# Both magnitude sums of the second expert's w2b ahead of tile 1's Relu, and 26 of 30 early w1a pieces beside the attention chunks

## What is computed

```python
# attention: B=4, H=8, S=768, D=64, gamma per head
state = gamma * state + k_t v_t^T
y_t = scale * q_t @ state
x = y as [3072, 512]
# soft MoE (phi, w1a, w2a): 4 slots per expert
logits = x @ phi
slot_in = softmax(logits, axis=0).T @ x
slot_out[e] = relu(slot_in[e] @ w1a[e]) @ w2a[e]
x = softmax(logits, axis=1) @ slot_out
# top-2 MoE (w_gate, w_noise, noise, w1b, w2b)
noisy = x @ w_gate + log1p(exp(x @ w_noise)) * noise
for each token, its two best experts e with weights p:
    out += p * relu(x @ w1b[e]) @ w2b[e]
```

## Time and profile before

| | us |
|---|---|
| median of 3 runs | 539.45 (538.11 to 540.13) |
| the profiled execution | 539.68 |
| its span | 537.8 |
| PE busy | 492.4 (92%) |
| DVE, ACT, POOL busy | 276.2, 185.8, 254.2 |

### The profile page before, as it was taken

One profiled execution on the slowest core, in us unless ns is written; L12 is line 12 of the kernel. 1 busy time (PEld: TensorE's weight loads), 2 busy tenths in 40 slices (PEclk: granted clock), 3 DMA queues, 4 the chain that ended last, 5 costly groups with the idle time before them and its releaser, 6 DMA issues.

```text
span 537.8 us, 13565 instructions
## 1 busy us (share of the span) xinstructions
PE 492.4 (92%) x4844; PEld 291.5 (54%) x4845; DVE 276.2 (51%) x443; ACT 185.8 (35%) x346; POOL 254.2 (47%) x217
## 2 busy tenths in 40 slices
PE   3999999987978667989999999999999999999995
PEld 3877787863567243444544544545545445445452
DVE  2676766666221897463646455464545332433422
ACT  0222222221003537665455363554442222223210
POOL 2222222202000024525777868786878766666553
PEclk9999999998997889999999999999999999999999
DMA  7999999989999999342466342132232332433410
GB/s 276 400 359 398 401 401 404 380 340 333 403 425 424 390 417 400 112 174 85 161 217 198 102 137 49 27 58 45 44 59 44 53 47 43 57 42 42 60 20 2
DMA packets 35096, 107.93 MB, mean 201 GB/s; under 512 B 11871, under 2 KB 13135, under 8 KB 32624
## 3 DMA queue, kind: packets, MB, share of 16 engines
q1 hardware_dynamic: 20880, 92.90, 44.6%
q0 software_dynamic: 14176, 14.49, 14.8%
HBM read 93.87 MB, written 29.43 MB: 229 GB/s over the span
## 4 chain that ended last, share of the span: by engine, by line
PE 76%; DMA 13%; DVE 3%; issue 3%; POOL 2%; ACT 1%; SPq 1%; DVEq 0%; POOLq 0%
PE ps L1019 47%; DMA w_region<-moe_w 7%; PE ps L1002 4%; PE ps L672 4%; PE ps L736 4%; DMA late_w1a<-chunks 4%; PE ps L856 3%; PE ps L885 3%; DMA out<-s_region,rec_region 2%; PE ps L712 2%; PE ps L726 2%; PE ps L747 2%; PE ps L686 1%; POOL out L625 1%; SPq L524 1%
## 5 line engine op out<-in xcount | busy, mean ns | idle before, releaser
L1019 PE MATMUL ps<-w_region,s_region 128*128 (+1 forms) x1304 | 290.4, 379 | 2.0 <-DVE s_region L1704 1.0
L1019 PEld LDWEIGHTS ps<-w_region,s_region 128*128 128x128 f16 x1304 | 125.4, 98 | 143.4 <-issue 2.8
L1674 DVE SCALAR_TENSOR_TENSOR s_region<-ps,s_region 128x1024 f16<-128x1024 f32 x55 | 67.3, 1224 | 144.2 <-ACT s_region L1232 144.1
L1232 ACT ACTIVATE s_region<-ps 128x1024 f16<-128x1024 f32 x55 | 56.3, 1024 | 176.5 <-PE ps L1002 176.5
L619 POOL DMA_INDIRECT out<-s_region,rec_region x41 | 53.9, 1315 | 49.4 <-DVE s_region L1704 46.1
L625 POOL DMA_INDIRECT out<-s_region,rec_region x42 | 66.9, 1593 | 19.2 <-issue 11.9
L613 POOL DMA_INDIRECT rec_region<-records,idx x55 | 60.1, 1092 | 24.4 <-issue 16.3
L559 POOL TENSOR_TENSOR s_region<-w_region,s_region 128x512 f32<-128x512 f32 x14 | 14.6, 1043 | 50.0 <-PE ps L747 31.9
L1002 PEld LDWEIGHTS ps<-s_region,sw_region 128*128 (+1 forms) x440 | 29.6, 98 | 14.0 <-issue 0.8
L1704 DVE TENSOR_SCALAR s_region<-ps,rec_region,y_scale 128x512 f32<-128x512 f32 x42 | 33.8, 805 | 5.9 <-PE ps L1019 4.1
L1002 PE MATMUL ps<-s_region,sw_region 128*128 128x128 f16 x440 | 34.5, 219 | 0.5 <-ACT s_region L1227 0.4
(11 more groups left out here) (249 smaller groups left out, 571.1 us busy)
## 6 DMA issues: line engine op xcount, KB each, us to landing
w_region<-moe_w SPq DMA_DIRECT2D x49, 512.0 KB, 11.2
w_region<-moe_w SPq DMA_DIRECT2D x10, 2048.0 KB, 8.7
w_region<-chunks SPq DMA_DIRECT2D x26, 512.0 KB, 7.2
s_region<-moe_w SPq DMA_DIRECT2D x4, 2048.0 KB, 12.9
sw_region<-chunks SPq DMA_DIRECT2D x12, 512.0 KB, 7.2
late_w1a<-chunks SPq DMA_DIRECT2D x8, 512.0 KB, 8.2
w_region<-moe_w SPq DMA_DIRECT2D x3, 1024.0 KB, 8.0
s_region<-moe_w SPq DMA_DIRECT2D x5, 512.0 KB, 8.4
```

What stands on the lines that cost most here:

```text
L1019: last = nc.tensor.matmul(bank[6 + r], h[:, r, f, :], w2b_parts[:, bass.ds(o, 1), part, f, :].rearrange("p e m -> p (e m)"), start=(first ...
L1232: nc.scalar.activation(h_hi[:, r, :, :].rearrange("p c t -> p (c t)").rearrange("p (a n) -> p a n", a=2), ps[:, 2 + 2 * r:4 + 2 * r, :], A ...
L1674: nc.vector.scalar_tensor_tensor(out=h_lo[:, r, :, :].rearrange("p c t -> p (c t)").rearrange("p (a n) -> p a n", a=2), in0=ps[:, 2 + 2 * ...
```

## The change

Two things are changed. First, only 26 pieces of w1a are issued beside the chunks. After chunk g there are g - 2 of them up to chunk 10, and from chunk 11 on one more for every third chunk. The other four (quarters 2 and 3 of expert 6, quarters 0 and 1 of expert 7) follow behind the noise, ahead of the wait for x_t, with a semaphore of their own, for which L856 waits at expert 6.

Second, both sums of the second expert's w2b follow each other on ACT, ahead of ct of tile 2 and the Relu of tile 1. The reduction stands on POOL after the sixth fetch, and the scale on DVE ahead of the low part and y of tile 1 and 0.

```diff
+        CHUNK_QUARTERS = EARLY_QUARTERS - 4
...
-                more = (g - 2) * EARLY_QUARTERS // (NT - 3)
+                more = g - 2 + max(0, g - 8) // 3
                 for q in range(ahead, more):
-                    w1a_quarter(q // 4, q % 4)
+                    w1a_quarter(q // 4, q % 4, w1a_early)
...
             sp.dma_start(noise_t, noise[:, :, :]).then_inc(noise_full, 16)
+            for q in range(CHUNK_QUARTERS, EARLY_QUARTERS):
+                w1a_quarter(q // 4, q % 4, w1a_late)
             sp.wait_ge(x_t_ready, NT)
...
-            for i in range(4, 2 * DEPTH + 3):
+            for i in range(4, DEPTH + 2):
+                fetch_records(i)
+            w2b_all_sum(EARLY)
+            for i in range(DEPTH + 2, 2 * DEPTH + 3):
                 fetch_records(i)
...
-                if i == 0:
-                    w2b_all_sum(EARLY)
...
-            pe.wait_ge(w1a_early, 16 * EARLY_QUARTERS)
+            pe.wait_ge(w1a_early, 16 * CHUNK_QUARTERS)
             for e in range(E):
+                if e == CHUNK_QUARTERS // 4:
+                    pe.wait_ge(w1a_late, 16 * (EARLY_QUARTERS - CHUNK_QUARTERS))
...
-            w2b_sum_part(EARLY, 0, junk)
             stage_c(2, 0, rec_arrival(2))
+            w2b_sums(EARLY, junk)
+            keep_ct(2, 0)
             h_high(1, 1)
-            keep_ct(2, 0)
             stage_c(3, 1, rec_arrival(3))
+            keep_ct(3, 1)
             h_high(2, 0)
-            keep_ct(3, 1)
-            w2b_sum_part(EARLY, 1, junk)
             w2b_high(EARLY)
...
-            low_keep(0, 0, None)
-            h_low(2, 0)
             w2b_scale_by_sum(EARLY)
             dve.wait_ge(order_ready, 1)
             scale_y(EARLY)
+            low_keep(0, 0, None)
+            h_low(2, 0)
             w2b_low(EARLY)
```

7 lines of the change are left out of this document (4 added, 3 removed).

## The result

| | us |
|---|---|
| before, median of 20 runs | 539.7 (536.6 to 541.59) |
| after, median of 20 runs | 542.55 (538.26 to 545.69) |
| ratio | 1.0051, 95% interval 1.0035 to 1.0067 |
| the profiled execution of after | 541.53, span 539.6 |

The change costs 2.8 us where 4.1 us of gain were forecast. The kernel after was timed twice more, each time against before on the same chip: 1.0021 (0.9989 to 1.005) and 1.005 (1.0013 to 1.0086). The profiled executions differ by 1.85 us (541.53 - 539.68). In the kernel after, lines ahead of the second MoE's tile loop are 5 to 7 higher (L1019 is L1026, L1476 is L1482, L1485 is L1491, L928 is L935, L856 is L863, L672 is L677), and on POOL 4 higher (L619 is L623, L625 is L629, L589 is L593).

A forecast was written before the change was run, and what follows sets the result against it. The prediction saw full DMA bounding the kernel until the last w1b piece, then PE in the tile loop. From the profiled 539.68 us, -3.0 (A) and -1.1 (B) gave 535.6, as a median 535.4; range 533.8 to 538.8.

The forecast's parts named there:

- Part A: Moving four w1a pieces behind the noise: fewer chunk waits and a filled DMA hole, -3.0 us, bounds -3.5 and -1.0.
- (a): Attention: with fewer w1a pieces ahead of the chunks, all 3.0 us of PE's avoidable chunk waits go, lower end 2.0.
- (c): Early attention, one piece per chunk: landings of 5.8 us stay above 3.2, so no new DMA idle time.
- (b): DMA at 119 to 128 us: four moved pieces (2.1 MB, 5.4 us) fill a hole of 3.2 us; L856 starts at 126.0.
- Rival (1): Front: the queue drains before chunk 10, up to 3.9 us idle replaces the hole's 3.2; 538.3 us, chance 0.14.
- Part B: Reordered start of the tiles: -0.55 at tile 3 and -0.55 at the second PE wait, -1.1 us, bounds -2.0 and +2.4.
- the first wait: PE's 0.99 us wait for y of tile 1 before tile 3, forecast to go: start at 234.5 instead of 235.01.
- The hold of POOL: POOL's DMAs slowed beside DVE's low halves of expert 1: at worst tile 1's rows go out 0.75 us later.
- rival (3): Tiles: POOL holds DVE, two waits of at most 1.6 us, y of tile 1 at 235.1; 536.0 us, chance 0.06.
- So ACT starts at 248.1 to 248.5: ACT on expert 2's high half starts 0.8 to 1.2 us earlier; PE waits about 0.5 us instead of 1.00.
- rival (2): Tile 0's rows land behind the w2b[3] load, expert 2's scale is late, PE loses 2.4 us; 538.8 us, chance 0.16.
- (5): Fuller DMA queues cause more untraced waits, read as code fetches, on DVE or PE; 541.0 us, slower, chance 0.07.

The follow-up runs named there:

- front_only: Only the w1a part of the change (26 pieces beside the chunks, four behind), tiles in the old order, against before: 546.33 us, ratio 1.002.
- tiles_sum2_w2b3_late: Before plus the new tile order, the third expert's w2b reduction ahead of tile 2's add, and w2b[3] loaded after tile 5's Relu: 536.89 us, 0.9933.
- tiles_sum2_early: Before plus the new tile order and the third expert's w2b reduction ahead of tile 2's add: 537.11 us, 0.9944; run again 537.64 us, 0.987.

## Why the prediction was wrong

**Part A, -3.0 forecast, -0.24 in the profile.** The reading of the waits was right: they went. But already here less came through than (a) took. L856 came 2.15 us sooner, and 1.09 of that is the first load, which the change leaves alone. The step that failed is (c), "I take no new idle time", together with the use of the hole as a gain in (b). Rival (1) has the outcome, the front regains nothing, but not the place: it looked for the loss before chunk 10 (whose piece is issued at 39.58 in after), and from 10 to 60 us both kernels moved 388 GB/s. So of the text's signs of being wrong, "below 380 GB/s between 10 and 60" did not show, and "the last w1b piece at 209 still" did. The arithmetic was at hand: 26 pieces instead of 30 leave 2.1 MB less to be moved during the attention, while the attention gets at most 3.0 us x 391 GB/s = 1.2 MB shorter. The rest, 0.9 MB or more, must show as a lower rate somewhere before 119, whatever the landings look like; measured were 1.53 MB. That the queue ran thin beside the later chunks follows from the bytes; the share of the DMA engines there (1.00 and 0.99) doesn't show it. The landings, on which (c) relied, did behave as it said; they say whether PE waits, not whether the queue is always full. Up to the last w1b piece the DMA counts and not the slots: with 128 to 217 us added, the kernels moved 81.1 MB (before) and 81.3 MB (after) from 10 to 217 us, 0.15 MB or 0.4 us apart, and PE took that piece 0.23 us earlier.

**Part B, -1.1 forecast, +2.0 in the profile.** Right: +0.45 for the start of the 40 matmuls (to the hundredth by luck, since the Relu of tile 1, which the text has at 221.0, began at 220.54 + 0.24 = 220.78 in the clock of before); the reduction at 220.57, near the 221.4 of the text in the clock of before; both sums at once without hurting PE; DVE in time for h_low and y of tile 0; y of tile 1 out at 232.0 (231.20 + 0.80; the text has 231.9 in the clock of before); the first wait gone. This first gain was even too small in the text: of the 1.94 us that PE was ahead at tile 6, 0.24 are the front's, and part B has 1.70, not 0.55. The small gap of 0.69 us ahead of tile 3, which the text did not count, went as well. The hold of POOL was right too: two DMAs beside L1482 took 2.13 and 2.55 us, where the others take 1.03 and 1.57. DVE was not held (4.60 us for two low halves, 4.61 before), so rival (3) did not come, and the rule of the Trainium skill that the prediction weighed against the trace holds for the POOL half alone again.

The step that failed is "So ACT starts at 248.1 to 248.5". It let the chain to expert 2's scale follow the load's issue (by the Relu of tile 3) and the y of tile 4, both of which did come earlier (DVE was done with y of tile 4 at 245.98 instead of 247.93, and then waited 2.67 us for POOL). The chain hangs on the landing of tile 1's write, and this one hung on the end of a 2.10 MB load, which was at 243.0 in both kernels although the load was issued 1.07 us sooner. ACT started at 249.42. The text named that load, and rival (2) was built on the same mechanism, but for tile 0's rows, and for the case that POOL came late. POOL was early, and it did not help: a write begun 0.35 us ahead of the load landed behind it all the same. The 0.86 us of front_only were enough, so that the write met the load at all may be the hold of POOL at work, which the text had named and priced at 0.75 us; no run takes the hold away.

The second failure is of the same size. The text priced a longer wait at its length alone. PE's clock fell during it, and 1.64 us went in the tile behind. So 1.94 us gained ahead of a fixed point did not come to zero, but to a loss of 1.76 us one tile later (258.58 against 256.82).

The +2.0 is that of one pair of profiles. Over the three pairs the tails of before are 315.7, 316.1 and 316.5 us and those of after 317.3, 317.0 and 317.1, on average 1.0 us longer; with the 0.45 ahead of them that is some 1.5 us (an estimate). The medians differ by 2.8, 1.3 and 3.1 us. What makes up the rest is not shown; a cost of the front is not excluded.

**The chances.** "Slower" had 0.07, for a cause (5) that the runs don't show. PE's waits with nothing to wait for in the first MoE are still there, 2.50 us at 159.20, and remained hidden. The closest rival for the whole was (2), but even it ended at 538.8, since it counted part A in full; without the 3.0 us of part A it is 541.8.

**What stays open.** Why the new order of the tiles alone was 0.9954 in the one comparison where before took 544.74. Before takes 544.7 to 545.9 us on two chips and 539.7 to 540.5 in three comparisons elsewhere, while the tiles with the early reduction take 537.1 and 537.6 on either kind. The stall of 3.67 us in front_only, with its half clock some 5 us, would be the difference if the old order always had it on those two chips. It was seen in one profile only, the comparison that was to tell came on a chip of the other kind, and what ACT waited for in it the trace doesn't say. Nor was it tried why the write lands behind a load that is issued 0.35 us after it has begun, when in front_only 0.86 us between them were enough. The Trainium skill (DMA: Bandwidth & Descriptors, Queues, rings and completion order) says that each DMA engine takes turns between its queues, a packet at a time. That alone doesn't give the 8.38 and 10.14 us that were measured, and no run here tells how the turns went.

**Better than both** are the versions with the new order of the tiles and the early reduction. tiles_sum2_w2b3_late took 536.89 us, 0.9933 of before, and tiles_sum2_early, whose edit is smaller, 0.9944 and 0.987.

## What to carry to other kernels

Before counting what an engine gains, find the next event that it meets and ask what fixes that event's time; a gain that ends at an event fixed by a transfer is lost, and if the longer wait lowers TensorE's clock, it costs more than it gave. Fill a hole in the DMA's time only with bytes that would otherwise move after it: bytes taken from before it leave the sum as it was, and the rate x time of both stretches, added up, tells so in advance. Where an engine's queue has a short step behind waits that are not its own, move the step ahead of them first; here it was worth 1.0 us in the old order of the tiles and 4.2 us in the new one.
